# One transfer with a three-dimensional address in place of four for each output tile of state rows

## The reference

```python
B, H, S, Ns, D = (8, 8, 512, 32, 64)
# attention: xread (B, H, 512, D) and sread (B, H, 32, D), joined along the rows
x = attn_out.transpose(0, 2, 1, 3).reshape(B * S, H * D)   # here S is 512 + 32 = 544
x = _moe_ref(x=x, **moe_kwargs)
h = x @ w_in                                               # (4352, 512) @ (512, 2048)
g = np.maximum(h, 0.0) + alpha * np.minimum(h, 0.0)
return g @ w_out                                           # (4352, 512), float32
```

## Time and profile before

| | |
|---|---|
| median of 3 runs | 1387.61 us (1387.15 to 1390.89) |
| the profiled execution | 1389.19 us |
| its span, first to last instruction | 1387.4 us |
| PE busy | 1334.0 us, 96% of the span |
| DVE, ACT, POOL busy | 825.6, 422.3, 175.7 us |
| stores of the output on SP | 40 issues: 32 of 256 KB, 8 of 64 KB |

### The profile page before, as it was taken

One profiled execution on the slowest core, in us unless ns is written; L12 is line 12 of the kernel. 1 busy time (PEld: TensorE's weight loads), 2 busy tenths in 40 slices (PEclk: granted clock), 3 DMA queues, 4 the chain that ended last, 5 costly groups with the idle time before them and its releaser, 6 DMA issues.

```text
span 1387.4 us, 22367 instructions
## 1 busy us (share of the span) xinstructions
PE 1334.0 (96%) x7773; PEld 1150.5 (83%) x7774; DVE 825.6 (60%) x1071; ACT 422.3 (30%) x609; POOL 175.7 (13%) x228
## 2 busy tenths in 40 slices
PE   8998599999989999996999999999999999999998
PEld 7877488888868888885899999999978888888886
DVE  6776652224555525256677776778976556666652
ACT  6886331112233313235121210212322222222221
POOL 3563022111212222222000000000000000000000
PEclk9999799999999999998999999999999999999999
DMA  7884371113456415343543334343344444444453
GB/s 273 272 285 138 93 233 72 45 38 106 166 192 239 163 71 179 120 162 90 207 139 128 120 129 145 130 144 137 133 122 125 122 116 113 113 113 113 116 120 52
DMA packets 180738, 193.40 MB, mean 139 GB/s; under 512 B 25313, under 2 KB 130785, under 8 KB 180193
## 3 DMA queue, kind: packets, MB, share of 16 engines
q1 hardware_dynamic: 173440, 172.51, 39.5%
q0 software_dynamic: 6112, 19.93, 4.2%
q10 hardware_dynamic: 1152, 0.56, 0.2%
HBM read 125.07 MB, written 67.37 MB: 139 GB/s over the span
## 4 chain that ended last, share of the span: by engine, by line
PE 92%; DVE 3%; ACT 2%; issue 1%; ACTq 0%; DMA 0%; DVEq 0%; POOL 0%; POOLq 0%
PE ps_p L377 13%; PE ps_p L379 13%; PE ps_p L378 13%; PE ps_y L377 5%; PE ps_y L379 5%; PE ps_h L377 5%; PE ps_y L378 5%; PE ps_h L379 5%; PE ps_h L378 5%; PE ps_o L379 5%; PE ps_o L377 5%; PE ps_o L378 5%; PE ps_hT L1536 2%; PE ps_sr L1413 1%; PE ps_xT L1530 1%
## 5 line engine op out<-in xcount | busy, mean ns | idle before, releaser
L377 PE MATMUL ps_p<-b_hi,w_hi 128*128 128x272 f32 x896 | 258.3, 288 | 4.1 <-DVE b_lo L1248 4.1
L379 PE MATMUL ps_p<-b_hi,w_lo 128*128 128x272 f32 x896 | 258.5, 289 | 0.0
L378 PE MATMUL ps_p<-b_lo,w_hi 128*128 128x272 f32 x896 | 258.5, 289 | 0.0
L377 PEld LDWEIGHTS ps_p<-b_hi,w_hi 128*128 128x128 f32 x896 | 168.6, 188 | 5.0 <-DVE b_lo L1248 5.0
L379 PEld LDWEIGHTS ps_p<-b_hi,w_lo 128*128 128x128 f32 x896 | 168.8, 188 | 0.0
L378 PEld LDWEIGHTS ps_p<-b_lo,w_hi 128*128 128x128 f32 x896 | 168.1, 188 | 0.0
L1181 DVE COPY hid<-ps_h 128x512 f32<-128x512 f32 x74 | 51.2, 691 | 135.2 <-PE ps_h L379 129.4
L377 PE MATMUL ps_h<-w_hi,xgT_hi 128*128 128x512 f32 x296 | 122.5, 414 | 7.3 <-DVE w_lo L961 5.5
L1183 DVE SCALAR_TENSOR_TENSOR hidT_lo<-ps_hT,hidT_hi 128x512 fp32r<-128x512 f32 x74 | 51.2, 692 | 121.1 <-ACT hidT_hi L841 121.1
L377 PE MATMUL ps_y<-w_hi,hidT_hi 128*128 128x512 f32 x296 | 122.7, 415 | 0.0
L841 ACT ACTIVATE hidT_hi<-ps_hT 128x512 fp32r<-128x512 f32 x74 | 44.3, 599 | 247.1 <-PE ps_hT L1536 247.1
(11 more groups left out here) (224 smaller groups left out, 2387.3 us busy)
## 6 DMA issues: line engine op xcount, KB each, us to landing
acts<-gb SPq DMA_DIRECT2D x128, 272.0 KB, 2.1
stage<-in_moe_w SPq DMA_DIRECT2D x32, 1024.0 KB
gt<-acts SPq DMA_DIRECT2D x32, 1024.0 KB, 6.1
xN_all<-in_xN SPq DMA_DIRECT2D x8, 1024.0 KB, 6.3
rows_x<-xrow SPq DMA_DIRECT2D x32, 256.0 KB, 2.7
out_rows<-orow SPq DMA_DIRECT2D x32, 256.0 KB, 2.0
yz<-rows_y SPq DMA_DIRECT2D x30, 256.0 KB, 3.1
xs_all<-in_xT SPq DMA_DIRECT2D x7, 1024.0 KB, 6.7
```

Source lines behind the costliest of these rows:

```text
L377: pe.matmul(out, s_hi, m_hi, start=start, stop=False)
L378: pe.matmul(out, s_hi, m_lo, start=False, stop=False)
L379: return pe.matmul(out, s_lo, m_hi, start=False, stop=stop)
```

## The change

The state rows of the output get a three-dimensional view, batch x row in the batch x column, cut to the last 32 rows of each batch. `store_tile` takes a piece of the output and not a list of first rows, and makes one transfer of it. For a token tile it is the same 128 neighbouring rows as before. For a state tile it is `of_state[4 * k:4 * k + 4]`, of the shape 4 x 32 x 512. The last wait asks for one completion for each state tile and not for four.

```diff
             def store_tile(t, k, rows):
                 wait_apart(sp, o_copied, t + 2 + 1)
-                n = P // len(rows)
-                for j, r in enumerate(rows):
-                    sp.dma_start(out_v[bass.ds(r, n), :], orow[j * n:(j + 1) * n, k % 2, :])\
-                      .then_inc(o_stored[k % 2], 16)
+                sp.dma_start(rows, orow[:, k % 2, :]).then_inc(o_stored[k % 2], 16)
+
+            of_state = out_v.rearrange("(b t) c -> b t c", t=TB)[:, S:TB, :]
...
-                    store_tile(t, k, [g * TB + k * P])
+                    store_tile(t, k, out_v[bass.ds(g * TB + k * P, P), :])
...
-                store_tile(t, k, [(B - 1) * TB + k * P])
+                store_tile(t, k, out_v[bass.ds((B - 1) * TB + k * P, P), :])
             for k in range(2):
-                store_tile(XT + k, k, [(4 * k + j) * TB + S for j in range(4)])
+                store_tile(XT + k, k, of_state[4 * k:4 * k + 4])
             for k in range(2):
-                sp.wait_ge(o_stored[k], 16 * (1 + XT // 2 + 4))
+                sp.wait_ge(o_stored[k], 16 * (1 + XT // 2 + 1))
```

## The result

| | before | changed |
|---|---|---|
| median of 22 runs each | 1389.51 us (1387.15 to 1390.89) | 1392.38 us (1390.00 to 1393.31) |
| span of the profiled execution | 1387.4 us | 1390.5 us |
| its time | 1389.19 us | 1392.34 us |

The ratio is 1.0021 with a 95% interval of 1.0015 to 1.0027: the change costs 2.9 us (2.1 to 3.8). That is less than 0.3%, and with 22 runs it is clearly not nothing.

The account below looks back on a forecast made before the run. TensorE's matmuls bound the kernel, with only the last store exposed. 1383.93 + 0.21 issue + 1.30 fixed + 3.5 data = 1388.94 landing, 2.0 us later in span; 1387.61 + 2.0 = 1389.6 us, range 1386.5 to 1391.5.

Parts of the forecast that it names:

- The place: End of program, tile 33's copy, stores and wait: only these 3.02 us can change; tile 32's store is covered by matmuls.
- The engines: Tile 33's merged store: outermost DRAM count 4 gives four engines, 132 packets with 4 small ones; chance 0.72.
- The rivals of 16 engines and of one: Merged store's engines: all 16, 1386.8 us, chance 0.20; one, 1397.3 us, chance 0.06 together with two engines.
- The sign and the sum: Tile 33's landing moves to 1388.94, span 1389.4: 2.0 us slower, bounds +1.3 and +2.8 us.
- Data: Tile 33's store: 32 packets one after another on each of four engines, 3.5 us, between 2.8 and 4.3.
- The upper price, 135 ns a packet: Packet cost read from the four old state stores; on four engines it gives 4.3 us of data.
- The rest: Tile 33's store apart from data: 0.21 us of extra issue and 1.30 us of fixed part.
- The last wait: SP's wait at the program's end: from 1.3 us to about 4.4 us, with 16 engines 1.6 us.
- the bounds that I gave for the mechanism: Prediction counted as wrong if SP's last wait is under 3.5 us or over 6 us.
- The level: Whole kernel's time: median of earlier runs, 1387.61 us, plus 2.0 gives 1389.6 us, range 1386.5 to 1391.5.
- Within 0.3%: Whole kernel's time: change of 0.14%, not to be told from no change; 0.90 for the same within 0.3%, about 4.2 us.

## Why the prediction was right or wrong

**The place** was right. The chain's end, matmul, copy, store, wait, is the only stretch that changed, and tile 32 is covered (the runs with one tile changed).

**The engines** were right: four small packets, and 16, 8 and 2 with other counts. The Trainium skill's rule ("DMA: Bandwidth & Descriptors", the section on the semaphore's 16) is borne out for all four: the largest number up to 16 that divides both slowest dimensions. All counts here were powers of two, so no run tells the largest divisor from the smaller count. The rivals of 16 engines and of one both fall for the shape of the change.

**The sign and the sum** were right in direction and short in size. Forecast was 2.0 us more, with bounds of 1.3 and 2.8; the profile shows 2.86, the runs 2.9. Two terms were mis-sized:

- Data: I took 3.5 us between 2.8 and 4.3. It measured 4.07 us for each engine, 0.57 more. The upper price, 135 ns a packet, was nearer the 127 measured, but for no reason that I gave. I had explained 135 ns by two engines at one port of SBUF, with the Trainium skill's "SBUF — State Buffer", section "Door 1", behind it, and by my price this would have slowed every packet. The packets behind the slow start take 84 ns, about as in a token tile's store (87), and the surplus is all in the slow start, 1.4 us for each engine, a term that my sum did not have. So for four engines that begin 32 rows apart no run shows a port conflict in the steady part; whether the slow start is one, no run tells.
- The rest: 0.21 + 1.30 = 1.51 us forecast, 5.88 - 4.07 = 1.81 measured. The issue's length was right (0.58 against 0.34 + 0.21 = 0.55), but the first packet also comes later, 1.2 us after the start of the issue and not 0.8 as in a token tile's store: unlike sides on 16 engines added 0.4 us to the landing, not 0.21. The four engines also don't end together; their small packets lie 0.6 us apart.

**The last wait** was forecast at 4.4 us and is 5.3, inside the bounds that I gave for the mechanism.

**The level** was wrong, and with it the range. The forecast of 1389.6 us stood on the median of three runs, 1387.61. Over 22 runs the same kernel has a median of 1389.51, 1.9 us more, and the profiled execution, 1389.19, had already been nearer to it. The measured 1392.38 lies 0.9 us above the range's end of 1391.5. From a base of 1389.5 the forecast would have been 1391.5, and of the 2.8 us between 1389.6 and 1392.38 two thirds are the base and one third the sum. The bounds of the sum, +1.3 and +2.8, would then have given 1390.8 to 1392.3, and the measured time is at their upper end. The step that failed is that of the scatter: the three runs lay at 1387.15, 1387.61 and 1390.89, and the range took their median as the base and added about one microsecond, where it needed the whole spread. The mis-sized terms of the sum, the data with its slow start above all, are the smaller part of the miss.

**Within 0.3%** was right as a size. That it could not be told from no change was not: 22 runs against 22 give an interval of 0.12%.

## What to carry to other kernels

Before several transfers are made into one, look at the outermost count of both sides as the program has it: fewer instructions with a small outermost count (4 here) can give three quarters of the DMA engines away, and it is paid in full where nothing covers the landing. Where matmuls lie over the store, the merged one cost no time here, but look at what is queued behind it: a load behind it landed 3 us later. Let the program end with the tile whose store is plainest. A forecast of a microsecond or two needs its base from many runs, and not from the median of three that scatter over twice as much, nor from one profiled execution, which scatters as they do; here that one was near by luck.

## What the runs showed of the hardware

- One transfer from SP ran on 16, 8, 4 or 2 engines for an outermost DRAM count of 32, 8, 4 or 2 against 128 or 64 rows of SBUF (16, 8, 4 and 2 small packets). Two transfers of 2 engines each ran on the same two (landing 7.8 us).
- On 2, 4 and 8 engines with 16 or more packets from 16 or more rows each, an engine's first packets of 2 KB took up to 0.47 to 0.92 us, where most later ones took 84 ns. On 16 engines with 8 rows each no packet took over 98 ns, with 8 packets each on 4 engines none over 165 ns.
- A load of 1 MB issued right behind a 256 KB store on four engines landed in 9.4 us; behind four stores of 64 KB on 16 engines it took 6.2 us.
- Unlike shapes of the two sides held SP 0.51 to 0.80 us for a store's issue against 0.34 us for a token tile's, and delayed the landing by 0.4 us in all (2.4 against 2.0 us for 256 KB on 16 engines).
